# Attention values brought back to rows: three transposes, a copy and two GpSimd steps against one product and one VectorE step

## The chip, the cores and the metric

One core of a Trainium2 chip. It has five engines with a queue each: TensorE (PE; its weight loads are listed apart, as PEld), VectorE (DVE), ScalarE (ACT), GpSimd (POOL) and SyncE (SP, which here issues most of the transfers). They meet through semaphores only: an instruction adds to one when it has finished, and another engine waits for a count. PE writes to PSUM, in 8 banks; DVE and ACT read PSUM and SBUF; POOL reads and writes SBUF only. The metric is the time of one execution on the device, in microseconds (us).

## The reference

Three parts in a row, all in float32, for 2 batches of 768 rows:

```python
q_bits, k_bits = (q @ proj > 0), (k @ proj > 0)          # 6 hash bits a row
mask = bucket(q_bits)[:, None] == bucket(k_bits)[None, :]
scores = np.where(mask, scale * q @ k.T, -1e9)
attn = np.exp(scores - scores.max(-1))
out = attn / (attn.sum(-1) + 1e-9) @ v                   # 16 heads (2 x 8), 768 x 64 each
x = heads side by side                                   # (2, 768, 512)

u = x + real(fft2(x)); un = layernorm(u)                 # first mixer
x = u + relu(un @ w_ch1) @ w_ch2

theta = x @ w_theta                                      # second mixer
u = x + w_tok_r @ (x * cos(theta)) + w_tok_i @ (x * sin(theta))
out = u + relu(u @ w_ch)
```

## The kernel before

Every float32 matrix product is made of three products of rounded parts (high x high, high x low, low x high), so each operand exists as a high part (type fp32r, written by ACT or POOL) and a low part (the difference, by DVE or POOL). The plain float32 tensors that PE sees are the ones it transposes.

**Attention** runs over 16 heads `h` (`NH`) and, in each, over six tiles of 128 query rows, t = 0 to 5 (`QT`). `schedule()` writes the order out by hand as a list of slots, one for each tile; every engine's block walks the same list and takes its own share of a slot, so the order on each engine is fixed and only semaphores place it in time. In the slot of tile n:

- PE makes the scores of tile n (L1006, L1007, into one of two double banks), transposes the exponentials E of tile n - 2 in two units `eta` and `etb` of three 128x128 transposes (L981), adds a third of the value products of a half head (`pv`, L1021 and L1022, into the one bank `OT`), and then makes the slot's extra units: `bits` (hash bits of the next head, t = 0 and 1) or `back` (t = 3 and 5, for the head before). The units `eta`, `etb`, `bits` and `back` take turns in a ring of three banks; `take_bank` waits until the unit three back has been emptied.
- DVE takes the maximum of the scores (`negmax`, L1237), makes scale and bias for the exponential from it (`affine`, L1240, 128x2), writes the two low parts `ETL` (L1247), and in the slot t = 3 makes the reciprocals of the row sums (`einv`, L1266 and L1268).
- ACT writes the high parts `ETH` (L768), the exponential `E` (L775), the copy `OS` of a finished half head out of `OT` (L787), and the copies of the extra units (`MB` for bits, `OL` for back).
- POOL runs freely behind its semaphores: `mask_rows` (MR, L562; slot t = 1, when ACT has copied both bits units), `scale_q` (QK, L547) and `split_top` (the copy TOPH, L555, and TOPL, L557; t = 2), `split_v` (VHL, L581 and L583; t = 4), some folds for the transform in the last heads, and `finish`.

What the change touches is the way of the values back to rows. `OS` holds a half head transposed: 64 partitions of products with the high part of v and 64 with the low part, for 3 x 128 rows. Before, a `back` unit transposes it in three 128x128 pieces into a ring bank (L992), ACT copies the bank to `OL2` (L800), and POOL's `finish` adds the two halves of 64 columns into `OS2` (L571) and multiplies by `einv` into the rows of X (L574), for the first half in slot t = 3 of the next head and for the second in t = 0 of the one after:

```python
nc.gpsimd.tensor_tensor(OS2[:], OL2[:, i, :, 0:D], OL2[:, i, :, D:P], ALU.add)
nc.gpsimd.tensor_tensor(X[:, row:row + HALF, (h % H) * D:(h % H + 1) * D], OS2[:], einv..., ALU.mult)
```

The semaphore `s_x` counts the halves of X written; the folds for the transform, the first loads of the feed-forward weights and DVE's `fold_sum` (AE, L1156) wait for it.

After attention come the transform of X by matrix products (`half_transform`, `cosine_part`, `sine_part`), the feed-forward part (`hidden` and `shrink`, 48 steps) and the second mixer (`steps`). Of these the change only touches waits on PE.

Of the kernel before, what the change touches and what calls it, by code (L numbers as in the profile page):

```python
# [84 lines left out]
def program(nc, qk, v, projb, w1, w2, wth, wtr, wti, wch, ident_in, gamma_in, sign_in, cs_in, ss_in, alt_in, cd_in, sd_in, out):  # L85
# [16 lines left out]
    X = put("X", [P, NT, DM])  # L102
    ident = put("ident", [P, P])
    negmax = put("negmax", [P, NSTAT, 2])
    affine = put("affine", [P, NSTAT, 2])
# [12 lines left out]
    halfpi = put("halfpi", [P, 1])  # L118
    tail = used[0] + 4 * 2 * DM
    OL2 = put("OL2", [P, 2, HALF, P], F32, tail - 4 * 2 * DM)  # L120
    OS2 = put("OS2", [P, HALF, D])
    used[0] = tail
    tail = used[0]
# [112 lines left out]
    with ctx:  # L236
# [39 lines left out]
        for u in units:  # L276
# [30 lines left out]
                   "pv": sem("s_os"),  # L307
                   "back": sem("s_ol")}
        s_sum = sem("s_sum")
        s_x = sem("s_x")  # L310
        s_mr = sem("s_mr")
# [144 lines left out]
        def _(sp):  # L456
# [38 lines left out]
            load_qk(1)  # L495
            sp.dma_start(ident[:], ident_in).then_inc(s_ident, 16)
            move_away(0)
# [38 lines left out]
        def _(pool):  # L536
# [22 lines left out]
            def mask_rows(h):  # L559
                pool.wait_ge(emptied["bits"], 2 * (h + 1))  # L560
                pool.wait_ge(s_mask, 32 * h)
                nc.gpsimd.tensor_scalar(MR[:], MB[:], gamma[:, 0:1], gamma[:, 1:2], ALU.is_gt, ALU.mult).then_inc(s_mr, 1)  # L562

            def finish(h, i):
                half = 2 * h + i
                st = slice((half * HALF) % NSTAT, (half * HALF) % NSTAT + HALF)
                row = (h // H) * QT + i * HALF
                pool.wait_ge(emptied["back"], half + 1)
                if half:
                    pool.wait_ge(s_x, half)  # L570
                nc.gpsimd.tensor_tensor(OS2[:], OL2[:, i, :, 0:D], OL2[:, i, :, D:P], ALU.add).then_inc(s_sum, 1)  # L571
                pool.wait_ge(s_sum, half + 1)
                pool.wait_ge(s_inv, 2 * (h + 1))
                nc.gpsimd.tensor_tensor(X[:, row:row + HALF, (h % H) * D:(h % H + 1) * D], OS2[:],  # L574
                                        einv[:, st].unsqueeze(2).to_broadcast([P, HALF, D]), ALU.mult).then_inc(s_x, 1)

# [65 lines left out]
            for slot, (tile, et, pv, us) in enumerate(slots):  # L642
                h, t = divmod(slot - 1, QT)
                if slot and t == 0:
                    if h == 0:
                        split_top(1)
                        split_v(0)
                    elif h > 1:
                        finish(h - 2, 1)
                if slot and t == 1 and h + 1 < NH:  # L650
                    mask_rows(h + 1)
                if slot and t == 2 and h + 2 < NH:
                    scale_q(h + 2)
                    split_top(h + 2)
                if slot and t == 3 and h:
                    finish(h - 1, 0)
                if slot and t == 4 and h + 1 < NH:
                    split_v(h + 1)
                if slot and t in (2, 5) and early:
                    dst, src, landed = early.pop(0)  # L660
                    pool.dma_start(dst, src).then_inc(landed, 16)
                if (h, t) in ((9, 5), (10, 5), (11, 5)):
                    fold_part(h - 9, False)
                if (h, t) in ((12, 5), (13, 5), (14, 1)):
                    fold_part(h - 12, True)
                if (h, t) == (14, 2):
                    fold_even(0)
                if (h, t) == (14, 5):
                    fold_odd(0)
                if (h, t) == (15, 1):  # L670
                    fold_even_low(0)
                if (h, t) == (15, 4):
                    fold_odd_low(0)
            finish(NH - 1, 1)
            fold_odd(1)
# [32 lines left out]
        def _(act):  # L708
# [50 lines left out]
            for slot, (tile, et, pv, us) in enumerate(slots):  # L759
# [28 lines left out]
                for u in us:  # L788
                    kind, h, i = u
                    c = slice(i * HC, (i + 1) * HC)  # L790
                    if kind == "bits" and h:
# [3 lines left out]
                        nc.scalar.activation(MB[:, c], ring(unit_no[u])[0:2 * NM, 0:HC], ACT.Copy).then_inc(emptied["bits"], 1)  # L795
                    elif kind == "back":
                        act.wait_ge(s_ring, done[u])
                        if h:
                            act.wait_ge(s_sum, nth[u] - 2)
                        nc.scalar.activation(OL2[:, i], blocks(ring(unit_no[u])[:, 0:HC]), ACT.Copy).then_inc(emptied["back"], 1)  # L800
                    elif kind == "s1" and i < TG - 1:
                        half_high(0, i)
# [84 lines left out]
        def _(pe):  # L887
# [81 lines left out]
            def unit(name):  # L969
# [4 lines left out]
                if kind in ("eta", "etb"):  # L974
                    tile = h * QT + i
                    pe.wait_ge(s_exp, tile + 1)
                    if tile == 0:
                        pe.wait_ge(s_ident, 16)
                    first = 0 if kind == "eta" else HALF
# [9 lines left out]
                elif kind == "back":  # L989
                    pe.wait_ge(emptied["pv"], 2 * h + i + 1)  # L990
                    for j in range(HALF):
                        last = nc.tensor.transpose(bank[:, j * P:(j + 1) * P], OS[:, i, j * P:(j + 1) * P], ident[:])  # L992
                last.then_inc(s_ring, 1)

            for tile, et, pv, us in slots:
                if tile is not None:
                    h, t = divmod(tile, QT)
                    pe.wait_ge(s_away, 32 * (h + 1))
                    pe.wait_ge(s_in, 32 * (h + 1))
                    pe.wait_ge(s_mask, 32 * (h + 1))  # L1000
                    if tile >= 2:
# [10 lines left out]
                if pv is not None:  # L1012
                    h, c, part = pv
                    if part == 0:
                        pe.wait_ge(s_vs, 2 * h + 2)
                        pe.wait_ge(emptied["eta"], h * QT + (c + 1) * HALF)
                        pe.wait_ge(emptied["etb"], h * QT + (c + 1) * HALF)
# [44 lines left out]
            def hidden(g):  # L1062
                c, f = divmod(g, FT)
                pe.wait_ge(s_uth, CH * (c + 1))
                pe.wait_ge(s_utl, CH * (c + 1))
                if g >= 2:
# [37 lines left out]
            def step(kind, n, t):  # L1104
# [6 lines left out]
                elif kind in ("theta", "channel"):  # L1111
                    y = xt_no[kind, n]
                    pe.wait_ge(s_xth, y + 1)
                    pe.wait_ge(s_xtl, y + 1)
                    pe.wait_ge(s_wlow, n_wth if kind == "theta" else n_wch)
                    take_turn(kind, n)
# [4 lines left out]
                elif kind == "mix":  # L1121
                    c = n % QT
                    pe.wait_ge(s_zl, 2 * (n + 1))
                    pe.wait_ge(s_wlow, n_wth + 2 * (c + 1))
                    if n == 0:
# [24 lines left out]
        def _(dve):  # L1150
# [80 lines left out]
            for slot, (tile, et, pv, us) in enumerate(slots):  # L1231
# [22 lines left out]
                for u in us:  # L1254
# [6 lines left out]
                    elif kind == "s1" and i < 2:  # L1261
                        half_low(0, i)
                    elif kind == "back" and i == 0:
                        st = slice(h * QT % NSTAT, h * QT % NSTAT + QT)
                        dve.wait_ge(s_exp, (h + 1) * QT)
                        nc.vector.tensor_scalar(einv[:, st], esum[:, st], 1e-9, None, ALU.add).then_inc(s_inv, 1)  # L1266
                        dve.wait_ge(s_inv, 2 * h + 1)
                        nc.vector.reciprocal(einv[:, st], einv[:, st]).then_inc(s_inv, 1)  # L1268

# [147 lines left out]
def constants():  # L1417
# [6 lines left out]
    def parts(a):  # L1424
# [5 lines left out]
    return {  # L1430
        "ident": np.eye(P, dtype=np.float32),
        "gamma": np.array([[0, 1]] * BITS + [[-TINY, 1]] * BITS + [[-TINY, -PEN]] * BITS + [[0, -PEN]] * BITS, dtype=np.float32),
# [48 lines left out]
```

## Time and profile before

| | |
|---|---|
| median of 3 runs | 743.95 us (743.7 to 744.09) |
| the profiled execution | 744.51 us, its span 742.7 us |
| PE (matmul) busy | 716.0 us, 96% |
| PE weight loads | 604.6 us, 81% |
| DVE busy | 427.9 us, 58% |
| ACT busy | 336.6 us, 45% |
| POOL busy | 322.8 us, 43% |
| granted TensorE clock | 1.0 of full speed |

The span runs from the first instruction to the last; the time has some 1.8 us around it. The ends of matmuls are modelled and overlap, so a busy PE is not yet a PE at its peak: what matters is whether one starts as the one before lets it. Shares over the whole span hide that the stages differ: DVE is nearly always busy in attention and mostly idle behind it.

### The profile page before, as it was taken

What the parts mean: (1) busy time and instruction counts of PE and PEld (TensorE: products, weight loads), DVE (VectorE), ACT (ScalarE), POOL (GpSimd) and SP (SyncE); (2) the same over time, 40 slices, a digit from 0 to 9 for tenths busy, and PEclk for the clock granted to TensorE, in tenths of its full rate; (3) what the DMA queues carried; (4) which work ended last, traced back from release to release, by engine and by line L of the source; (5) the groups of instructions that cost most, each with busy time, mean ns of one, the idle gap of its engine ahead of it and who ended that gap; (6) DMA issues with size and microseconds to landing.
All of it is one profiled execution on the core that took longest, in us unless ns stands there. A gap on an engine that the chain in (4) does not pass through costs nothing.

```text
span 742.7 us, 10815 instructions
## 1 busy us (share of the span) xinstructions
PE 716.0 (96%) x3754; PEld 604.6 (81%) x3754; DVE 427.9 (58%) x731; ACT 336.6 (45%) x689; POOL 322.8 (43%) x284
## 2 busy tenths in 40 slices
PE   3999999999998999999999999999999999999998
PEld 2788888888887877788888888888888888888876
DVE  2899999999999777733122121211333556845443
ACT  1899989988987834433210111121223344123101
POOL 3688878878887339855100000020033564221100
PEclk9999999999999999999999999999999999999999
DMA  6464753444332012423000000110011210000002
GB/s 162 117 146 113 176 146 84 99 113 100 88 73 66 1 44 64 135 85 100 0 1 1 0 1 2 41 57 22 1 42 44 85 50 29 1 28 15 15 28 86
DMA packets 39399, 45.76 MB, mean 62 GB/s; under 512 B 15796, under 2 KB 26676, under 8 KB 39348
## 3 DMA queue, kind: packets, MB, share of 16 engines
q1 hardware_dynamic: 36564, 41.65, 20.5%
q0 software_dynamic: 2784, 3.43, 1.8%
q8 instruction: 32, 0.52, 0.3%
q14 instruction: 19, 0.16, 0.1%
HBM read 28.16 MB, written 3.15 MB: 42 GB/s over the span
## 4 chain that ended last, share of the span: by engine, by line
PE 76%; DVE 15%; issue 4%; ACT 2%; DMA 1%; POOL 1%; SPq 0%; ACTq 0%; POOLq 0%; DVEq 0%
PE PS L890 21%; PE PS L892 21%; PE PS L891 21%; DVE negmax L1237 6%; DVE ETL L1247 4%; DVE affine L1240 3%; PE PS L1021 2%; PE PS L981 2%; PE PS L1007 2%; PE PS L1006 2%; PE PS L1022 2%; PE PS L1109 1%; ACT OS L787 1%; PE PS L1036 1%; PE PS L992 1%
## 5 line engine op out<-in xcount | busy, mean ns | idle before, releaser
L1390 DVE SCALAR_TENSOR_TENSOR HL<-PS,HH 128x512 fp32r<-128x512 f32 x48 | 33.1, 691 | 154.7 <-ACT HH L876 154.7
L775 ACT ACTIVATE E<-PS,affine 128x768 f32<-128x768 f32 x96 | 95.2, 992 | 38.8 <-DVE affine L1240 36.1
L876 ACT ACTIVATE HH<-PS 128x512 fp32r<-128x512 f32 x48 | 28.7, 598 | 180.9 <-PE PS L892 180.9
L1237 DVE TENSOR_REDUCE negmax<-PS 128x1 f32<-128x768 f32 x96 | 90.8, 946 | 16.9 <-PE PS L1007 15.8
L1247 DVE TENSOR_TENSOR ETL<-PS,ETH 128x384 fp32r<-128x384 f32 x192 | 97.0, 545 | 2.5 <-ACT ETH L768 2.5
L981 PE MATMUL PS<-ident,E 128*128 128x128 f32 x576 | 81.8, 275 | 2.2 <-DVE ETL L1247 2.1
L768 ACT ACTIVATE ETH<-PS 128x384 fp32r<-128x384 f32 x192 | 82.7, 486 | 0.9 <-PE PS L981 0.8
L1021 PE MATMUL PS<-ETH,VHL 128*128 128x384 f32 x192 | 72.3, 377 | 5.2 <-ACT OS L787 4.7
L890 PE MATMUL PS<-UTH,W 128*128 128x512 f32 x192 | 75.8, 395 | 0.2 <-issue 0.2
L1006 PE MATMUL PS<-TOPH,TOPL 128*128 128x512 f32 x192 | 69.1, 360 | 6.5 <-DMA KM<-MR 6.2
L892 PE MATMUL PS<-UTH,W 128*128 128x512 f32 x192 | 74.8, 390 | 0.0
L891 PE MATMUL PS<-UTL,W 128*128 128x512 f32 x192 | 74.8, 389 | 0.0
L892 PE MATMUL PS<-W2H,HL 128*128 128x512 f32 x192 | 74.7, 389 | 0.0
L890 PE MATMUL PS<-W2H,HH 128*128 128x512 f32 x192 | 74.7, 389 | 0.0
L891 PE MATMUL PS<-W2L,HH 128*128 128x512 f32 x192 | 74.7, 389 | 0.0
L981 PEld LDWEIGHTS PS<-ident,E 128*128 128x128 f32 x576 | 65.4, 141 | 6.0 <-DVE ETL L1247 4.7
L1022 PE MATMUL PS<-ETL,VHL 128*128 128x384 f32 x192 | 64.7, 337 | 0.0
L693 POOL TENSOR_TENSOR WAL<-SRC,WAH 128x512 fp32r<-128x512 f32 x4 | 5.1, 1282 | 136.8 <-ACT WAH L852 136.8
L1007 PE MATMUL PS<-KM,QM 76*128 76x512 f32 x192 | 62.8, 347 | 0.0
L702 POOL TENSOR_TENSOR ZF<-X,SC 128x512 f32<-128x512 f32 x24 | 30.5, 1294 | 71.1 <-ACT SC L857 71.1
L562 POOL TENSOR_SCALAR MR<-MB,gamma 24x768 fp32r<-24x768 f32 x15 | 44.0, 2931 | 38.4 <-ACT MB L795 38.4
L890 PE MATMUL PS<-ZH,WTH 128*128 128x512 f32 x144 | 57.5, 400 | 0.0
(173 smaller groups left out, 1572.2 us busy)
## 6 DMA issues: line engine op xcount, KB each, us to landing
RAW<-in_moe_w_ch_dram SPq DMA_DIRECT2D x32, 256.0 KB, 2.7
QK<-in_qk_dram SPq DMA_DIRECT2D x16, 384.0 KB, 3.8
QM<-TOPH SPq DMA_DIRECT2D x16, 192.0 KB, 2.9
KM<-TOPL SPq DMA_DIRECT2D x16, 192.0 KB, 3.2
VR<-in_v_dram SPq DMA_DIRECT2D x16, 192.0 KB, 2.7
TOPL<-QM SPq DMA_DIRECT2D x16, 192.0 KB, 2.7
TOPH<-TOPH SPq DMA_DIRECT2D x16, 192.0 KB, 3.0
out_dram<-fin SPq DMA_DIRECT2D x12, 256.0 KB, 2.0
```

The source lines that it names most:

```text
L768: nc.scalar.activation(ETH[:, t // HALF, k * HALF:(k + 1) * HALF, (t % HALF) * P:(t % HALF + 1) * P], bank, ACT.Copy).then_inc(s_eth, 1)
L775: nc.scalar.activation(E[:, tile % NE, :], s_bank(tile)[:, 0:S], ACT.Exp, bias=affine[:, t, 1:2], scale=affine[:, t, 0:1], accum_out=esum[ ...
L890: nc.tensor.matmul(dst, hl, hr, start=start, stop=False)
L891: nc.tensor.matmul(dst, hl, lr, start=False, stop=False)
L892: return nc.tensor.matmul(dst, ll, hr, start=False, stop=stop)
L981: last = nc.tensor.transpose(bank[:, j * P:(j + 1) * P], E[:, tile % NE, (first + j) * P:(first + j + 1) * P], ident[:])
L1006: nc.tensor.matmul(dst, TOPL[:, h % 3, c], TOPH[:, h % 3, lo:hi], start=True, stop=False)
L1007: last = nc.tensor.matmul(dst, QM[:, h % 2, c], KM[:, h % 2, lo:hi], start=False, stop=True)
L1021: nc.tensor.matmul(OT, VHL[:, h % 2, j, :], ETH[:, c, j, :], start=(j == 0), stop=False)
L1022: last = nc.tensor.matmul(OT, VHL[:, h % 2, j, :], ETL[:, c, j, :], start=False, stop=(j == QT - 1))
L1237: nc.vector.tensor_reduce(negmax[:, t, 1:2], s_bank(tile)[:, 0:S], AX_X, ALU.max, negate=True).then_inc(s_max, 1)
L1247: nc.vector.tensor_tensor(ETL[where], blocks(ring(unit_no[kind, h, t])[:, 0:HC]), ETH[where].bitcast(F32), ALU.subtract).then_inc(emptied[ ...
```

## The change

- `ident` gets a companion `twins`, 128x64, two 64x64 identities on top of each other (one more load at the start, from columns 128 to 191 of the same constant).
- A `back` unit is three products of a piece of OS (128x128, as the weights) with `twins` (64 columns), which bring the piece back and add its two halves in one; all in plain float32.
- DVE multiplies the 3 x 64 columns in PSUM by `einv` straight into X, in the slot of the unit, for the first half behind the reciprocal. ACT's copy to `OL2` and POOL's `finish` go, and their semaphores; the ring bank is free when DVE has written X (`s_x` is now `emptied["back"]`).
- Waits of PE that repeat one already passed are dropped: per tile, per value group, per feed-forward step, per mixer step.

```diff
     ident = put("ident", [P, P])
+    twins = put("twins", [P, D])
     negmax = put("negmax", [P, NSTAT, 2])
...
                    "pv": sem("s_os"),
-                   "back": sem("s_ol")}
-        s_sum = sem("s_sum")
-        s_x = sem("s_x")
+                   "back": sem("s_x")}
+        s_x = emptied["back"]
         s_mr = sem("s_mr")
...
             load_qk(1)
-            sp.dma_start(ident[:], ident_in).then_inc(s_ident, 16)
+            sp.dma_start(ident[:], ident_in[:, 0:P]).then_inc(s_ident, 16)
+            sp.dma_start(twins[:], ident_in[:, P:P + D]).then_inc(s_ident, 16)
             move_away(0)
...
 
-            def finish(h, i):
-                half = 2 * h + i
-                st = slice((half * HALF) % NSTAT, (half * HALF) % NSTAT + HALF)
-                row = (h // H) * QT + i * HALF
-                pool.wait_ge(emptied["back"], half + 1)
-                if half:
-                    pool.wait_ge(s_x, half)
-                nc.gpsimd.tensor_tensor(OS2[:], OL2[:, i, :, 0:D], OL2[:, i, :, D:P], ALU.add).then_inc(s_sum, 1)
-                pool.wait_ge(s_sum, half + 1)
-                pool.wait_ge(s_inv, 2 * (h + 1))
-                nc.gpsimd.tensor_tensor(X[:, row:row + HALF, (h % H) * D:(h % H + 1) * D], OS2[:],
-                                        einv[:, st].unsqueeze(2).to_broadcast([P, HALF, D]), ALU.mult).then_inc(s_x, 1)
-
             def split_v(h):
...
                         nc.scalar.activation(MB[:, c], ring(unit_no[u])[0:2 * NM, 0:HC], ACT.Copy).then_inc(emptied["bits"], 1)
-                    elif kind == "back":
-                        act.wait_ge(s_ring, done[u])
-                        if h:
-                            act.wait_ge(s_sum, nth[u] - 2)
-                        nc.scalar.activation(OL2[:, i], blocks(ring(unit_no[u])[:, 0:HC]), ACT.Copy).then_inc(emptied["back"], 1)
                     elif kind == "s1" and i < TG - 1:
...
                     tile = h * QT + i
-                    pe.wait_ge(s_exp, tile + 1)
+                    if kind == "eta":
+                        pe.wait_ge(s_exp, tile + 1)
                     if tile == 0:
-                        pe.wait_ge(s_ident, 16)
+                        pe.wait_ge(s_ident, 16 * 2)
                     first = 0 if kind == "eta" else HALF
...
                     for j in range(HALF):
-                        last = nc.tensor.transpose(bank[:, j * P:(j + 1) * P], OS[:, i, j * P:(j + 1) * P], ident[:])
+                        last = nc.tensor.matmul(bank[:, j * D:(j + 1) * D], OS[:, i, j * P:(j + 1) * P], twins[:], start=True, stop=True)
                 last.then_inc(s_ring, 1)
 
             for tile, et, pv, us in slots:
                 if tile is not None:
                     h, t = divmod(tile, QT)
-                    pe.wait_ge(s_away, 32 * (h + 1))
-                    pe.wait_ge(s_in, 32 * (h + 1))
-                    pe.wait_ge(s_mask, 32 * (h + 1))
+                    if t == 0:
+                        pe.wait_ge(s_away, 32 * (h + 1))
+                        pe.wait_ge(s_in, 32 * (h + 1))
+                        pe.wait_ge(s_mask, 32 * (h + 1))
                     if tile >= 2:
...
                     if part == 0:
-                        pe.wait_ge(s_vs, 2 * h + 2)
-                        pe.wait_ge(emptied["eta"], h * QT + (c + 1) * HALF)
+                        if c == 0:
+                            pe.wait_ge(s_vs, 2 * h + 2)
                         pe.wait_ge(emptied["etb"], h * QT + (c + 1) * HALF)
...
                 c, f = divmod(g, FT)
-                pe.wait_ge(s_uth, CH * (c + 1))
-                pe.wait_ge(s_utl, CH * (c + 1))
+                if f == 0:
+                    pe.wait_ge(s_uth, CH * (c + 1))
+                    pe.wait_ge(s_utl, CH * (c + 1))
                 if g >= 2:
...
                     c = n % QT
-                    pe.wait_ge(s_zl, 2 * (n + 1))
-                    pe.wait_ge(s_wlow, n_wth + 2 * (c + 1))
+                    if t == (CH if n == 0 else 0):
+                        pe.wait_ge(s_zl, 2 * (n + 1))
+                        if n < QT:
+                            pe.wait_ge(s_wlow, n_wth + 2 * (c + 1))
                     if n == 0:
...
                         half_low(0, i)
-                    elif kind == "back" and i == 0:
-                        st = slice(h * QT % NSTAT, h * QT % NSTAT + QT)
-                        dve.wait_ge(s_exp, (h + 1) * QT)
-                        nc.vector.tensor_scalar(einv[:, st], esum[:, st], 1e-9, None, ALU.add).then_inc(s_inv, 1)
-                        dve.wait_ge(s_inv, 2 * h + 1)
-                        nc.vector.reciprocal(einv[:, st], einv[:, st]).then_inc(s_inv, 1)
+                    elif kind == "back":
+                        if i == 0:
+                            st = slice(h * QT % NSTAT, h * QT % NSTAT + QT)
+                            dve.wait_ge(s_exp, (h + 1) * QT)
+                            nc.vector.tensor_scalar(einv[:, st], esum[:, st], 1e-9, None, ALU.add).then_inc(s_inv, 1)
+                            dve.wait_ge(s_inv, 2 * h + 1)
+                            nc.vector.reciprocal(einv[:, st], einv[:, st]).then_inc(s_inv, 1)
+                            dve.wait_ge(s_inv, 2 * h + 2)
+                        half = h * QT + i * HALF
+                        st = slice(half % NSTAT, half % NSTAT + HALF)
+                        row = (h // H) * QT + i * HALF
+                        dve.wait_ge(s_ring, done[u])
+                        nc.vector.tensor_tensor(X[:, row:row + HALF, (h % H) * D:(h % H + 1) * D],
+                                                ring(unit_no[u])[:, 0:HALF * D].rearrange("p (a b) -> p a b", b=D),
+                                                einv[:, st].unsqueeze(2).to_broadcast([P, HALF, D]), ALU.mult).then_inc(s_x, 1)
 
...
     return {
-        "ident": np.eye(P, dtype=np.float32),
+        "ident": np.concatenate([np.eye(P), np.tile(np.eye(D), (2, 1))], axis=1).astype(np.float32),
         "gamma": np.array([[0, 1]] * BITS + [[-TINY, 1]] * BITS + [[-TINY, -PEN]] * BITS + [[0, -PEN]] * BITS, dtype=np.float32),
```

## Rows read from the trace of the kernel before

**Rows 1.** busy time by stage: stretch, length, each engine's busy us (instructions)

```profile
30.11:221.87 191.76, 188.27 (x1246) 169.84 (x1245) 181.44 (x339) 172.68 (x391) 158.75 (x143) 1.00 0.46 116
221.87:268.34 46.47, 42.53 (x263) 36.16 (x261) 36.29 (x66) 33.12 (x76) 23.49 (x27) 1.00 0.15 39
268.34:742.70 474.36, 468.67 (x2176) 386.69 (x2176) 196.06 (x302) 118.42 (x202) 125.04 (x96) 1.00 0.12 37
```

**Rows 2.** chain of waits in one head: start us, us, what

```profile
116.34 0.41 PE PS L1021
...
117.28 0.33 PE PS L992 x3
...
118.33 0.66 PE PS L981 x6
...
123.55 0.97 DVE negmax L1237
...
124.54 0.52 DVE affine L1240
125.06 0.93 DVE ETL L1247 x2
...
129.15 0.17 DVE affine L1240
...
130.43 0.39 ACT OS L787
...
130.95 0.41 PE PS L1021
```

**Rows 3.** timeline of POOL, 123.5 to 131.5 us: start us, us, engine, line, operation

```profile
124.08 2.93 POOL L562 TENSOR_SCALAR MR<-MB,gamma 24x768 fp32r<-24x768 f32 x1 [2.92 <-ACT MB L795]
126.99 2.13 POOL L547 TENSOR_SCALAR QK<-QK 64x768 f32<-64x768 f32 x1
129.19 0.82 POOL L555 CAST TOPH<-QK 128x768 fp32r<-128x768 f32 x1
130.09 1.83 POOL L557 TENSOR_TENSOR TOPL<-QK,TOPH 128x768 fp32r<-128x768 f32 x1
```

**Rows 4.** timeline of DVE in the same stretch

```profile
128.09 0.19 DVE L1268 RECIPROCAL einv<-einv 128x6 f32<-128x6 f32 x1
128.20 0.92 DVE L1237 TENSOR_REDUCE negmax<-PS 128x1 f32<-128x768 f32 x1
```

**Rows 5.** timeline of DVE, 59 to 62.5 us

```profile
60.42 0.42 DVE L1240 SCALAR_TENSOR_TENSOR affine<-negmax 128x2 f32<-128x2 f32 x1
```

**Rows 6.** timeline of POOL in the same stretch

```profile
60.31 0.51 POOL L581 CAST VHL<-VR 128x384 fp32r<-128x384 f32 x1
```

**Rows 7.** timeline of DVE, 104 to 107.5 us

```profile
107.01 0.49 DVE L1240 SCALAR_TENSOR_TENSOR affine<-negmax 128x2 f32<-128x2 f32 x1
```

**Rows 8.** timeline of POOL, 103 to 108 us

```profile
106.97 0.51 POOL L574 TENSOR_TENSOR X<-OS,einv 128x192 f32<-128x192 f32 x1
```

**Rows 9.** groups by line, 20 to 272 us: busy us, mean ns | idle before

```profile
L1247 DVE TENSOR_TENSOR ETL<-PS,ETH 128x384 fp32r<-128x384 f32 x192 | 97.0, 545 | 2.5 <-ACT ETH L768 2.5
...
L571 POOL TENSOR_TENSOR OS<-OL 128x192 f32<-128x192 f32 x32 | 19.2, 601 | 16.5 <-ACT OL L800 11.2 <-DVE einv L1268 5.0
...
L574 POOL TENSOR_TENSOR X<-OS,einv 128x192 f32<-128x192 f32 x32 | 16.3, 510 | 2.5
...
L992 PEld LDWEIGHTS PS<-ident,OS 128*128 128x128 f32 x96 | 12.4, 140 | 1.1
```

**Rows 10.** timeline of DVE, 295 to 299 us

```profile
296.92 0.41 DVE L1211 TENSOR_TENSOR DS<-PS,BS 128x257 f32<-128x257 f32 x1
297.25 0.41 DVE L1212 TENSOR_TENSOR DS<-PS,BS 128x257 f32<-128x257 f32 x1
```

**Rows 11.** timeline of DVE, end of attention

```profile
265.97 1.76 DVE L1156 TENSOR_TENSOR AE<-X 128x1536 f32<-128x1536 f32 x1 [1.18 <-POOL X L574]
```

**Rows 12.** timeline of PE, end of attention

```profile
268.34 0.42 PE L890 MATMUL PS<-SSH,OH 128*127 128x386 f32 x1 [0.63 <-DVE TL L1204]
```

More of the change, by code:

```diff
@@ L118, in program @@
     halfpi = put("halfpi", [P, 1])
[L119 to L122, printed above, removed]
+    used[0] += 4 * 2 * DM
     tail = used[0]
@@ L647, in _ @@
                         split_v(0)
-                    elif h > 1:
-                        finish(h - 2, 1)
                 if slot and t == 1 and h + 1 < NH:
@@ L654, in _ @@
                     split_top(h + 2)
-                if slot and t == 3 and h:
-                    finish(h - 1, 0)
                 if slot and t == 4 and h + 1 < NH:
@@ L673, in _ @@
                     fold_odd_low(0)
-            finish(NH - 1, 1)
             fold_odd(1)
@@ L1114, in step @@
                     pe.wait_ge(s_xtl, y + 1)
-                    pe.wait_ge(s_wlow, n_wth if kind == "theta" else n_wch)
+                    if n == 0:
+                        pe.wait_ge(s_wlow, n_wth if kind == "theta" else n_wch)
                     take_turn(kind, n)
```

## The prediction

> **What bounds the kernel now.** I read the stages first, then the chain of waits inside one head, then the two engines that the change shifts work between.
>
> The stages [rows 1]: the 13 heads from 30.11 to 221.87 us take 191.76 us, 14.75 each; the last two heads and the run out of attention take 46.47; the transform, the feed-forward part and the second mixer take 474.36, of which PE is busy 468.67. In the third stretch PE is fed without gaps, so a wait that is dropped there was over when PE came to it. The attention heads are the place to look: PE busy 188.27 and DVE 181.44 of 191.76, POOL 158.75.
>
> There the chain of waits alternates [rows 2]. From 116.34 to 123.55 it runs on PE alone: one group of value products, one "back" unit (three transposes, 0.33), then scores, transposes and value products of the next tiles. From 123.55 to 129.32 it runs on DVE alone, tile t=2 to t=4 of the head: maximum, affine, two ETL pieces, and again, with the two small einv operations between. The affine of t=4 then releases the exponential on ACT, ACT copies OS at 130.43, and PE, which has only one bank OT for value products, goes on at 130.95. So a head is 14.61 here, and whatever is put on DVE between t=2 and t=4 is paid in full; PE and ACT have no part of it that could hide it.
>
> The same stretch on POOL [rows 3] and DVE [rows 4] shows what DVE waits for. The affine at 124.54 is 0.52 long instead of 0.16 and ends 0.98 after POOL began MR at 124.08. The next ones are free, and the one of t=4 starts at 129.15, 0.04 before POOL begins its copy into TOPH at 129.19. Both engines are timed from the start of MR (POOL runs MR, QK, TOPH, TOPL without a gap; DVE runs on from the release of the affine), so this phase repeats in nearly every head. What the copy does to an affine that comes later can be read elsewhere [rows 5, 6]: the affine at 60.42 met a POOL copy of the same kind (CAST, 60.31 to 60.82) and ended at 60.84, held to the copy's end. An affine at 107.01 met the multiplication into X and was held to 107.50 [rows 7, 8]. Heads with that hold are longer than 14.61; over the 13 heads such holds cost 191.76 - 13 x 14.61 = 1.8 us.
>
> **What the change removes.** POOL loses OS and X, 32 x (0.601 + 0.510) = 35.5 us [rows 9]. POOL is not what ends the wait in a head: MR waits 2.92 us for ACT [rows 3], and the operations behind MR are chained to MR. What comes back are the holds by these operations on the affine, the 1.8 us above. ACT loses the 32 copies into OL; before the affine of t=4 ACT is waiting anyway, so nothing comes back. The repeated waits on PE: in the PE stretch the groups follow each other without a gap [rows 2], in the last stage too [rows 1]: nothing. If they do cost something there, PE's idle of 191.76 - 188.27 = 3.5 us bounds it.
>
> **What it adds on PE.** A "back" unit becomes three products with 64 columns instead of three transposes with 128. No plain f32 product is in this trace. Below: half the columns of the transposes, 0.16 a unit. Above: each product done as two, each with a load of its own at the pace of a transpose (0.66 / 6 = 0.11, [rows 2]), 0.66 a unit. The weights loaded are the same 128x128 OS as before, with loads of 140 ns [rows 9]; I stay with that row, 0.33, no change. Only one of the head's two units is in the PE stretch (the other, in slot t=3, runs while DVE sets the pace), so the ends are 14 x (-0.17) = -2.4 and 14 x 0.33 = +4.6 us. The Trainium skill (FP8 and Floating Point Precision, TensorE Precision Notes) says that a true FP32 product takes four passes; no row here shows it, and by it 64 columns at 2.4 GHz would be 0.107 us a product, an estimate that leaves the unit at 0.32 and the sum as it is.
>
> **What it adds on DVE.** 32 multiplications, 128x192, one operand in PSUM and einv from SBUF. Nearest rows: the DS operations (257 elements, PSUM and SBUF) start 0.33 apart [rows 10], two ETL pieces of 384 take 0.93, 0.465 each [rows 2]; the line through both gives 0.27 for 192. In slot t=3 it comes behind the reciprocal and now waits for it: today the maximum starts at 128.20, inside the reciprocal's 128.09 to 128.28 [rows 4]; the multiplication can start at 128.30 and the maximum at 128.57. That is 0.37 later. The product that it reads was done long before. (The one in slot t=5 falls where DVE waits for PE's scores: nothing.) The ETL pieces average 545 ns over 192 [rows 9], the time of one that runs free, so an operation with one operand in PSUM is not held by POOL; I take the multiplication as not held either.
>
> **What is late next.** The affine of t=4 would start at 129.52 instead of 129.15. It then falls into the copy into TOPH, 129.19 to 130.01 [rows 3], and by [rows 5, 6] ends just behind it, at 130.03, instead of 129.31: 0.72 late, twice what was added. Exponential, OS copy and PE follow it, so the head becomes 14.61 + 0.72 = 15.33. POOL's TOPL from 130.09 holds the affine of t=5 to about the same time as before, and behind it PE sets the pace again, so nothing more is added.
> Which part of a POOL instruction holds the affine decides this. MR, 2.93 long, let it go after 0.98 [rows 2, 3]; the CAST kept it to its end. The Trainium skill (SBUF — State Buffer, Who interferes with whom) says that a DVE instruction with two SBUF inputs contends with a GpSimd one that reads SBUF, and that the one that comes first has the shared ports for the whole instruction. By that rule the copy holds the affine as the CAST row has it, and the sum is the one below; MR's row does not agree with it, and by MR's row alone the copy would let the affine through (the second rival).
>
> **The sum.** 13 heads: 13 x 15.33 - 191.76 = +7.5 (the holds that go away are in it). The end: the last X now comes from DVE instead of ACT and POOL; today DVE's AE waits 1.18 for it and PE then 0.63 for a TL behind it [rows 11, 12]; PE gets the 0.63 back, -0.6. The last two heads: POOL's folds run earlier without the X work and meet other affines, and two multiplications are added. Ends: -3.9 (all of PE's idle there, 46.47 - 42.53 [rows 1]) and +2.6 (2 x 0.37 and one hold as long as TOPL's 1.83 [rows 3]); I take 0 between them. Start: the second table load is issued in SP's idle time before the first move, nothing. Together +6.9, on the profiled execution's 744.51 (span 742.7 and 1.8 around it) 751.4; the runs' median is 743.95, 0.56 below it, so 750.9.
>
> **Rivals.**
> 1. The forecast with a dear product: 0.66 a unit on PE, 4.6 more, 755.5. For it: nothing in the trace shows an f32 product. Against: the same loads, half the columns.
> 2. The copy into TOPH holds only at its start, as MR does (0.98 / 2.93 of 0.82 is 0.27; the affine comes 0.33 in). Then a head is 14.61 + 0.37 and 13 x 14.98 - 191.76 - 0.6 = +2.4: 746.4. Against it stands the CAST row.
> 3. The other side: MR comes earlier. If the OL copies taken from ACT let MB, and so MR, start 0.9 earlier against DVE, the affine of t=2 is free (0.36 back, which pays the multiplication), the copy into TOPH is over when the affine of t=4 comes, a head is 14.61 and 13 x 14.61 - 191.76 - 0.6 = -2.4: 741.5. It decides from 0.9 us on; against it, ACT's MB follows an exponential that follows PE's scores, and the copy taken away lies a tile earlier.
> 4. The held affine of t=4 loses to TOPL as well (130.09 to 131.92): 1.9 more a head, +25, 776. Against: the gap of 0.08 between them, in which a waiting instruction is first.
>
> **How the numbers follow.** The forecast with a product at up to about 0.5 has 0.50, rival 1 0.13, rival 2 0.17, rival 3 0.09, rival 4 0.05; 0.06 is for what I don't see, spread over all signs. What a measurement here can tell from no change is about 0.2%, 1.5 us. Faster: rival 3 and a little, 0.11. Same: the low part of rival 2 (with the product's low end) and a little, 0.08. Slower: 0.81. The range takes the forecast with the ends of the product and of the last heads (748 to 754), rival 1 and most of rival 2: 745 to 757.
>
> **What would show it.** DVE: 32 multiplications near 0.35; the affine of t=4 near 0.5, ending with the copy into TOPH; affines of t=0 and t=1 near 0.16. Heads near 15.3 apart. PE: "back" units near 0.33, and longer waits for the OS copy. POOL some 35 us less busy, ACT 15. No change behind 300 us but the shift. Wrong would make it: an affine of t=4 that stays at 0.16, MR that starts earlier against the maximum of t=2, a product above 0.2 each, or a multiplication that POOL holds.

## The result, and the profile after

The changed kernel takes 760.7 us (median; 760.21 to 761.39), the kernel before 743.92 beside it: ratio 1.0225, 95% interval 1.0213 to 1.0237. It is slower by 16.8 us; 750.9 was forecast, in a range from 745 to 757 that does not hold it. The profiled execution has a span of 758.6 us (before 742.7).

The stages, in the form of [rows 1]: stretch, length, then each engine's busy us (instructions) in the order PE, PEld, DVE, ACT, POOL, then the granted clock and, last, the DMA engines' busy share and GB/s.

```profile
29.70:233.13 203.43, 195.99 (x1324) 179.51 (x1323) 178.18 (x365) 166.18 (x366) 133.88 (x96) 1.00 0.44 110
233.13:284.26 51.13, 47.38 (x280) 41.49 (x279) 38.39 (x72) 30.71 (x66) 13.77 (x10) 0.93 0.12 34
284.26:758.60 474.34, 468.68 (x2177) 386.67 (x2176) 196.07 (x302) 118.88 (x203) 125.05 (x96) 1.00 0.12 37
```

The 13 heads are 11.67 longer (203.43 against 191.76), the last two heads with the run out of attention 4.66 (51.13 against 46.47), the rest is as long as before, and the start is 0.41 shorter. That is 15.9, the whole difference of the spans.

The chain of waits in one head of the changed kernel, as in [rows 2] (start us, us, what):

```profile
128.77 0.97 DVE negmax L1218
...
129.77 0.51 DVE affine L1221
130.27 0.93 DVE ETL L1228 x2
...
133.53 0.36 DVE X L1256
133.89 0.88 DVE negmax L1218
...
134.79 0.46 DVE affine L1221
...
136.35 0.39 ACT OS L767
...
136.88 0.41 PE PS L998
...
137.82 0.61 PE PS L968 x6
138.43 0.29 PE PS L983
```

The stretch on DVE, from the maximum of t=2 to the end of the affine of t=4, took 5.77 before (123.55 to 129.32) and takes 6.48 (128.77 to 135.25): the multiplication (L1256) is in it, and the affine of t=4 is 0.46 long instead of 0.17. Behind OS, the three products of a unit (L968, six records) take 0.61 where the three transposes took 0.33 [rows 2], and the first score product behind them 0.29 where it took 0.24. Its line of the kernel before, in the same chain:

```profile
117.61 0.24 PE PS L1006
```

The timeline of POOL beside it, as in [rows 3], shows what the affine waited for: it ended at 135.25, just behind the copy into TOPH (134.40 + 0.82 = 135.22).

```profile
129.29 2.93 POOL L560 TENSOR_SCALAR MR<-MB,gamma 24x768 fp32r<-24x768 f32 x1 [6.24 <-ACT MB L775]
...
134.40 0.82 POOL L553 CAST TOPH<-QK 128x768 fp32r<-128x768 f32 x1
135.31 1.84 POOL L555 TENSOR_TENSOR TOPL<-QK,TOPH 128x768 fp32r<-128x768 f32 x1
```

Groups by line, 20 to 290 us, as in [rows 9] (busy us, mean ns | idle before): each product is two loads and two matmuls (32 units x 3 products = 96, in 192 records), and the multiplication takes 357 ns.

```profile
L968 PEld LDWEIGHTS PS<-twins,OS 128*128 128x128 f32 x192 | 26.6, 194 | 0.0
L968 PE MATMUL PS<-twins,OS 128*128 128x64 f32 x192 | 25.4, 269 | 0.0
...
L1256 DVE TENSOR_TENSOR X<-PS,einv 128x192 f32<-128x192 f32 x32 | 11.4, 357 | 6.1 <-PE PS L968 5.6
```

At the end of attention DVE's AE no longer waits, as it did in [rows 11]; the timeline of DVE:

```profile
281.14 0.35 DVE L1256 TENSOR_TENSOR X<-PS,einv 128x192 f32<-128x192 f32 x1
281.62 1.76 DVE L1137 TENSOR_TENSOR AE<-X 128x1536 f32<-128x1536 f32 x1
```

In head 14 something else happens. PE alone, one microsecond a row: stretch, length, busy us (records), granted clock, DMA.

```profile
246.00:247.00 1.00, 0.32 (x3) 1.00 0.55 163
247.00:248.00 1.00, 0.46 (x3) 1.00 0.02 8
248.00:249.00 1.00, 0.43 (x3) 1.00 0.00 0
249.00:250.00 1.00, 1.00 (x7) 0.68 0.00 0
250.00:251.00 1.00, 1.00 (x5) 0.50 0.00 0
...
255.00:256.00 1.00, 1.00 (x5) 0.50 0.00 0
256.00:257.00 1.00, 1.00 (x9) 0.90 0.00 0
```

For three microseconds PE is idle more than half of the time; then the granted clock falls from 1.00 to 0.50 (2.4 to 1.2 GHz) until some 256. Ahead of it DVE was held twice by POOL's folds (timelines of DVE, then of POOL; an affine or an einv that nothing holds takes 0.16). The first of these holds, in slot 3, was there before as well and as long (1.00), with the clock at 1.00 throughout:

```profile
242.04 1.00 DVE L1221 SCALAR_TENSOR_TENSOR affine<-negmax 128x2 f32<-128x2 f32 x1
...
243.90 1.11 DVE L1248 TENSOR_SCALAR einv<-esum 128x6 f32<-128x6 f32 x1
```

```profile
241.76 1.26 POOL L575 TENSOR_TENSOR AO<-X 128x512 f32<-128x512 f32 x1
243.16 1.81 POOL L579 TENSOR_TENSOR FE<-AE 128x765 f32<-128x765 f32 x1
```

### The profile page after: what moved, and what is told of

Same layout as the page of the kernel before. It is cut to its first block, busy times and chain, and to the rows that moved or that the text cites. A ratio compares the mean times of both kernels' runs of the same rounds, so it can differ in the third digit from the quotient of the medians.

```text
span 758.6 us, 10450 instructions
## 1 busy us (share of the span) xinstructions
PE 728.7 (96%) x3850; PEld 619.7 (82%) x3850; DVE 426.8 (56%) x763; ACT 328.1 (43%) x657; POOL 288.1 (38%) x220
## 4 chain that ended last, share of the span: by engine, by line
PE 79%; DVE 15%; issue 3%; ACT 1%; DMA 1%; SPq 0%; ACTq 0%; DVEq 0%
PE PS L865 21%; PE PS L867 21%; PE PS L866 20%; DVE negmax L1218 6%; DVE ETL L1228 4%; PE PS L998 3%; DVE affine L1221 3%; PE PS L957 3%; PE PS L983 3%; PE PS L984 2%; PE PS L999 2%; PE PS L968 1%; PE PS L1087 1%; ACT OS L767 1%; DVE X L1256 1%
```

## The experiments

One table first, to which each experiment refers. It cuts each profiled span in four: to the first maximum of head 1, from there to the first maximum of head 14, on to DVE's AE, and the rest. Each row is one profiled execution; the median is that of all runs. The period of a head is the time from its first maximum to that of the next.

```
                                   start  heads 1-13  to AE   rest    span   median
before                             30.11    191.76    44.10  476.73  742.7   743.92
changed                            29.70    203.43    48.49  476.98  758.6   760.7
e1 waits dropped, else before      29.31    191.71    44.11  476.77  741.9   744.7
e2 changed, with transposes        30.24    199.03    44.61  476.72  750.6   754.24
e3 before, with the products       30.00    203.46    44.79  476.95  755.2   756.93
e4 changed, query split first      29.56    206.51    45.61  477.02  758.7   760.41
e5 changed, unit in slot 4         29.86    192.26    43.47  477.01  742.6   744.37
e6 changed, folds late             29.28    203.30    44.76  477.06  754.4   757.21
e7 before, unit in slot 4          29.38    189.91    43.16  476.75  739.2   741.13
e8 e7 with folds late              29.42    189.86    43.82  476.80  739.9   742.05
e9 e5 with folds late              30.09    192.25    43.77  477.09  743.2   744.67
e10 e5 with rounded products       29.23    189.60    42.78  476.79  738.4   740.92
```

The medians of the kernel before that stand beside the experiments are 744.09 to 744.38, and the ratios are taken against those. The start lies between 29.23 and 30.24 with no order by kernel, the rest between 476.72 and 477.09. The first stretch is therefore not read.

**e1, the dropped waits alone, on the kernel before.** Edits of this kind at six places; one of them:

```diff
-                    pe.wait_ge(s_away, 32 * (h + 1))
-                    pe.wait_ge(s_in, 32 * (h + 1))
-                    pe.wait_ge(s_mask, 32 * (h + 1))
+                    if t == 0:
+                        pe.wait_ge(s_away, 32 * (h + 1))
+                        pe.wait_ge(s_in, 32 * (h + 1))
+                        pe.wait_ge(s_mask, 32 * (h + 1))
```

> The kernel before with the repeated waits of PE dropped and nothing else. Theory: a wait on a count that was reached long ago costs nothing that the trace shows, so the median stays at 743.9 within 0.2% (742.5 to 745.4). Rival: the waits cost PE's issue something in the long stages, and dropping them gains 1.5 or more; then the change hides a gain and its other parts cost more than the 16.8 by which it is slower.

Measured: 744.7, ratio 1.0005 (0.9996 to 1.0014); heads, last heads and the rest are within 0.1 of before. The waits cost nothing that can be measured (0.14% at most), and the change hides no gain in them.

**e2, the changed kernel with transposes.**

```diff
-  last = nc.tensor.matmul(bank[:, j * D:(j + 1) * D], OS[:, i, j * P:(j + 1) * P], twins[:], start=True, stop=True)
+  last = nc.tensor.transpose(bank[:, j * P:(j + 1) * P], OS[:, i, j * P:(j + 1) * P], ident[:])
...
-  ring(unit_no[u])[:, 0:HALF * D].rearrange("p (a b) -> p a b", b=D),
+  blocks(ring(unit_no[u])[:, 0:HC])[:, :, 0:D],
```

> The changed kernel with the three transposes of 128x128 in place of the three products with the twins; VectorE multiplies the high 64 columns of each block alone, so the low half of the value products is left out of the sum. Theory (the products are dear: a unit's three take 0.61 on the chain and the scores behind them 0.05 more, against 0.33 for the transposes): each head of 1 to 13 loses 0.34, so the period goes from 15.66 to about 15.32, 13 heads give back about 4.4, and with the last heads the time is 755 to 757. Rival (the products are hidden and the collision of the affine with the POOL copy is all of the 1.05 a head): the time stays at 760.7 within 1.5.

Measured: 754.24, ratio 1.0141 (1.0121 to 1.0161), a little under the expected range. The heads are 15.30 to 15.35 apart, as the theory had it, and 4.40 shorter than the changed kernel's; they are still 7.27 longer than before. The rival is out. The rest of the gain is in the last heads, 3.88: the profiled execution kept its clock there, though PE's idle before that is much the same as in the changed kernel:

```profile
242.00:243.00 1.00, 0.45 (x4) 1.00 0.62 185
243.00:244.00 1.00, 0.33 (x3) 1.00 0.02 8
244.00:245.00 1.00, 0.43 (x3) 1.00 0.00 0
245.00:246.00 1.00, 1.00 (x8) 1.00 0.00 0
```

The folds hold DVE in it as they do in the changed kernel: slots 3 and 4 of head 14, from maximum to maximum, are 4.48 and 2.31 long against 4.47 and 2.33. Only behind them do the two differ, in the last slot of head 14 (2.82 against 4.40) and the first of head 15 (2.08 against 3.85), which is 3.35 of the 3.88. Some 0.33 of it is the product in the last slot; the other 3.0, by that estimate, is what PE loses at 0.50. Of e2's four runs two have spans of 750.6 and 750.7 (mean clock 0.999 and 1.000) and two 753.1 and 753.3 (0.998). e4 below has such idle too (PE busy 0.26, 0.54 and 0.43 from 249 to 252) and keeps 1.00 there. Such idle therefore goes with a fall in some executions and not in others.

**e3, the products alone, on the kernel before.** PE as in the change; ScalarE copies the sums, POOL only multiplies:

```diff
-  last = nc.tensor.transpose(bank[:, j * P:(j + 1) * P], OS[:, i, j * P:(j + 1) * P], ident[:])
+  last = nc.tensor.matmul(bank[:, j * D:(j + 1) * D], OS[:, i, j * P:(j + 1) * P], twins[:], start=True, stop=True)
...
-  nc.gpsimd.tensor_tensor(OS2[:], OL2[:, i, :, 0:D], OL2[:, i, :, D:P], ALU.add).then_inc(s_sum, 1)
```

> The kernel before with the product with the twins alone: ScalarE copies the 192 columns to SBUF as before and POOL multiplies as before, but no longer adds; VectorE is given nothing new. Theory (the product costs 0.33 a unit on the chain that sets the head's period): 13 heads by 0.34 is +4.4, less what POOL's missing additions give back to the affines, so 746 to 749. Rival (the product is dear only together with the multiplication on VectorE): 743.9 within 1.

Measured: 756.93, ratio 1.0169 (1.0155 to 1.0183), outside both expectations. The heads take 203.46, as long as with the whole change, although DVE has no multiplication. The timelines of DVE and of POOL in head 7 show what holds it:

```profile
134.89 0.67 DVE L1238 SCALAR_TENSOR_TENSOR affine<-negmax 128x2 f32<-128x2 f32 x1
```

```profile
134.73 0.82 POOL L555 CAST TOPH<-QK 128x768 fp32r<-128x768 f32 x1
```

The affine of t=4 comes 0.16 behind the start of the copy (slot 3 of this head is 2.44 long, 2.28 to 2.29 before: the maximum of t=4 now waits for its scores, which PE makes behind the product) and is held for 0.67. The sum of slots 3 and 4 (from the maximum of t=3 to that of t=5) is 4.95 to 5.00 in the changed kernel, in e2 and in e3, against 4.24 or 4.25 before: the affine's end is pinned to the end of the copy, whatever made it late. So either half of the change alone costs some 0.72 a head here, and both cost it once; the product's 0.33 in slot 5 (3.14 against 2.81) comes on top wherever there is a product.

**e4, the query of head h+2 split ahead of the mask rows.**

```diff
-                if slot and t == 1 and h + 1 < NH:
-                    mask_rows(h + 1)
-                if slot and t == 2 and h + 2 < NH:
-                    scale_q(h + 2)
-                    split_top(h + 2)
+                if slot and t == 1:
+                    if h and h + 2 < NH:
+                        scale_q(h + 2)
+                        split_top(h + 2)
+                    if h + 1 < NH:
+                        mask_rows(h + 1)
```

> The changed kernel with POOL's scaling and splitting of the query of head h+2 issued ahead of the mask rows of head h+1, so that the copy into TOPH is over before the affine of slot 4. Theory (the affine of slot 4 is held to the end of that copy, mean 0.456 where 0.16 is the free price): the period falls by 0.30, from 15.66 to about 15.36, and the time to about 756.8, if the copy and the difference behind it don't hold the affines of slots 1 and 2 instead. Rival (the length of the affine is hidden, and the period is PE's): the period stays at 15.66 and the time at 760.7.

Measured: 760.41, ratio 1.0216 (1.0202 to 1.023). Both are right in part. The affine of t=4 is free in heads 1 to 13 (0.16), and heads 10 to 13 have a period of 15.39 to 15.43, as expected. But in heads 7 to 9 the copy's successor TOPL now holds the affine of t=0 (timelines of DVE and of POOL), those heads are 16.3 long; heads 1 and 2 take 17.41 and 16.85, with the clock at 0.50 from about 46 to 49. Why DVE and PE stand still ahead of that fall was not followed. The collision was moved, not removed.

```profile
126.47 1.62 DVE L1225 SCALAR_TENSOR_TENSOR affine<-negmax 128x2 f32<-128x2 f32 x1
```

```profile
126.23 1.84 POOL L555 TENSOR_TENSOR TOPL<-QK,TOPH 128x768 fp32r<-128x768 f32 x1
```

**e5, the changed kernel with the first half's unit a slot later.**

```diff
-        if h and t in (3, 5):
-            units.append(("back", h - 1, t // 5))
+        if h and t in (4, 5):
+            units.append(("back", h - 1, t - 4))
```

> The changed kernel with the first half's unit brought back in slot 4 instead of slot 3, so that the reciprocals (0.30) and the multiplication (0.36) come behind the affine of slot 4 and that affine runs before POOL's copy into TOPH. Theory (the stretch of VectorE from slot 2 to the affine of slot 4 sets the head together with PE): the period falls from 15.66 by 0.30 for the held affine and up to 0.66 for what leaves the stretch, less what the product now adds in slot 4: 14.9 to 15.3, so 750 to 756. Rival (PE's own work of two products is the bound once they are there): the period stays within 0.1 of 15.66, and the time at 759 to 761.

Measured: 744.37, ratio 1.0006 (0.9996 to 1.0015): with one slot changed the whole loss is gone, more than the theory gave (750 to 756, and a period of 14.9 to 15.3, not 14.80). The affine of t=4 starts before the copy into TOPH and is 0.16 long again (timelines of DVE and of POOL), and PE, with two dear units in slots 4 and 5, is never idle in these heads (stretches, columns as above):

```profile
128.98 0.16 DVE L1221 SCALAR_TENSOR_TENSOR affine<-negmax 128x2 f32<-128x2 f32 x1
```

```profile
129.28 0.82 POOL L553 CAST TOPH<-QK 128x768 fp32r<-128x768 f32 x1
```

```profile
30.00:120.00 90.00, 90.00 (x620) 83.76 (x619) 82.91 (x171) 78.24 (x173) 64.12 (x49) 1.00 0.58 140
120.00:220.00 100.00, 100.00 (x690) 93.52 (x689) 92.57 (x190) 86.77 (x191) 66.91 (x44) 1.00 0.38 95
```

Its period, 14.80 to 14.82 from head 2 on, is thus PE's own work with the products. On the chain two units take 2 x 0.33 more than two of transposes; but e7 below, with transposes in these slots, is only 0.2 a head shorter.

**e6, the changed kernel with two folds of head 14 later.**

```diff
-                if (h, t) in ((12, 5), (13, 5), (14, 1)):
+                if (h, t) in ((12, 5), (13, 5), (14, 5)):
                     fold_part(h - 12, True)
-                if (h, t) == (14, 2):
-                    fold_even(0)
                 if (h, t) == (14, 5):
+                    fold_even(0)
                     fold_odd(0)
```

> The changed kernel with POOL's two folds of head 14 issued behind the split of the last head's values, so that they no longer hold VectorE's affine and reciprocals in slots 3 and 4 of that head. Theory (PE stands idle there because VectorE is held, and the granted clock, 0.69 from 250 to 260 in the changed kernel, falls after that): the clock stays at 1.00 and the last two heads lose 2.5 to 4.5, so 756 to 758.2. Rival (the clock falls for another reason, or the folds hold something later instead): 760.7 within 1.5.

Measured: 757.21, ratio 1.0175 (1.016 to 1.019), as the theory had it. The stretch from head 14 to AE goes from 48.49 to 44.76, and the clock is 1.00 in it.

```profile
240.00:260.00 20.00, 17.32 (x116) 15.60 (x114) 18.71 (x33) 15.24 (x34) 11.34 (x9) 1.00 0.12 31
```

**e7 and e8, the kernel before with the unit in slot 4, and with the folds late too.** The edits of e5, and of e5 and e6, on the kernel before.

> The kernel before with the first half's unit and its reciprocals in slot 4 instead of slot 3. Theory (VectorE's stretch from slot 2 to the affine of slot 4 sets the head): it is 0.30 shorter without the reciprocals, and 13 heads give 739 to 742. Rival (the reciprocals only move to the next stretch, which is just as tight, or TOPL's difference holds slot 5's affine longer): 743.9 within 1.5, or slower.

Measured: 741.13, ratio 0.9964 (0.9951 to 0.9977). The heads lose 1.85 rather than 13 x 0.30: the period is 14.53 to 14.62 in ten of them, and the chain through head 7 now runs on PE almost without a break (PE busy 188.66 of the 189 us from 30 to 219, 185.81 before). With DVE's stretch shorter, PE is next; its transposes of E take up to 0.86 a six there instead of 0.66, and what holds them was not followed.

> The kernel before with the first half's unit in slot 4 and with POOL's two folds of head 14 behind the split of the last head's values. Theory: the folds held slot 3's affine of head 14 for 1.00 instead of 0.16 and made that head 17.65 long against 14.6 to 14.9 for the others; 1 to 3 of it come back on top of the first edit: 736 to 741. Rival (the folds then hold the last head instead): the same as the first edit alone.

Measured: 742.05, ratio 0.9974 (0.9963 to 0.9985): the rival. Head 14 is 14.48 instead of 15.72, and the last head gives it back: the folds hold its affines of t=0 and t=2 (1.30 and 1.19), and the clock falls behind an idle of PE (PE alone, one microsecond a row):

```profile
239.00:240.00 1.00, 0.00 (x0) 1.00 0.00 0
240.00:241.00 1.00, 0.55 (x3) 1.00 0.00 0
241.00:242.00 1.00, 0.45 (x3) 1.00 0.00 0
242.00:243.00 1.00, 1.00 (x4) 0.50 0.00 0
```

**e9 and e10, on the kernel of e5.** e9 adds the late folds. e10 has the products on fp32r operands:

```diff
-    OS = put("OS", [P, 2, HC])
+    OS = put("OS", [P, 2, HC], F32R)
...
+                    nc.gpsimd.tensor_copy(twinsR[:], twins[:]).then_inc(s_ident, 1)
...
-  OS[:, i, j * P:(j + 1) * P], twins[:], start=True, stop=True)
+  OS[:, i, j * P:(j + 1) * P], twinsR[:], start=True, stop=True)
```

> The changed kernel with both edits tried one at a time before: the first half's unit in slot 4, and POOL's two folds of head 14 behind the split of the last head's values. In the kernel with the unit in slot 4 alone TensorE is busy all the time in heads 2 to 13 (period 14.80) and head 14 takes 16.46. Theory: head 14 comes down towards 14.8 and 1 to 2 are gained: 742.5 to 743.5. Rival: the folds hold the last head instead, as they did in the kernel before with both edits, and the time stays at 744.4 or rises.

Measured: 744.67, ratio 1.0009 (1.0 to 1.0019): the rival again. Head 14 is 16.73 (16.46 in e5); the folds hold the affine of slot 5 instead (1.68).

> The changed kernel with the unit in slot 4 and with the products of the twins on operands rounded to fp32r (ScalarE writes OS in fp32r and the twins are copied into an fp32r tile once), so the value products lose their low bits before they are turned. Theory: the price of a product is that an fp32 one is run as two loads and two matmuls (3 products are 6 records of each kind); as one of each, a unit takes about half of 0.61, TensorE's need of a head falls from 14.80 by 0.5 to 0.6, and with what VectorE's stretch then leaves the period is 14.3 to 14.6: 737 to 741. Rival: the loads of the 128x128 blocks set the price whatever their type is split into, and the period stays at 14.80: 744.4 within 1.

Measured: 740.92, ratio 0.9955 (0.9938 to 0.9972), in the range of the theory: one load and one matmul a product (groups by line), 0.25 a unit on the chain instead of 0.61, and a period of 14.48 to 14.72. The first score product behind the unit takes 0.32, though, not 0.24 (chain of waits), so a unit with it costs 0.57, as much as one of transposes (0.33 + 0.24), and 0.90 with plain f32 (0.61 + 0.29). e7, e8 and e10 are the versions that beat the kernel before; e10 pays with the low bits of the value products.

```profile
L974 PEld LDWEIGHTS PS<-twinsR,OS 128*128 128x128 f32 x96 | 15.1, 189 | 0.1
L974 PE MATMUL PS<-twinsR,OS 128*128 128x64 f32 x96 | 13.3, 248 | 0.0
```

```profile
126.88 0.25 PE PS L974 x3
127.13 0.32 PE PS L989
```

## Why the prediction was wrong

**The bound and the mechanism in the heads were right.** The heads are set by the chain that alternates between PE and DVE, the multiplication lies in it between t=2 and t=4, and the affine of t=4 then falls into the copy into TOPH and is held to its end. The affine of t=4 is 0.40 later against the maximum of t=3 (slot 3 is 2.68 long, 2.28 or 2.29 before; 0.37 forecast), of which the multiplication is 0.36 (0.27 forecast; the line through its two rows gives 0.26). It is held to the end of the copy in all 13 heads, and in e2, which has this half of the change without the product, the heads are 7.27 longer; +7.5 was the forecast. Rival 2 (the copy holds only at its start) and rival 4 (TOPL holds too) are out in the changed kernel, rival 3 (MR earlier) as well: in head 7 MR starts 0.48 before the affine of t=2 (129.29 and 129.77), in the kernel before 0.46 [rows 2, 3].

**The step that failed first is the product's term.** "I stay with that row, 0.33, no change", from the loads of the transposes [rows 9]. A unit takes 0.61, and the scores behind it 0.05 more: 0.66, the upper bound and the price of rival 1. Against e2 it costs the heads 203.43 - 199.03 = 4.40, which is 13 x 0.34; the bound said 14 x 0.33. The heads are thus those of rival 1, which had 0.13; its 755.5 still lacks the next step. A load of the f32 product is 194 ns long, not the 140 of [rows 9], and there are two for each product. The row of the transposes was the nearest by its tile, not by what PE does with it. The Trainium skill (FP8 and Floating Point Precision, TensorE Precision Notes) says four passes for true FP32; the trace shows two loads and two matmuls for each product and 0.61 / 3 = 0.20 us, not the 0.107 that was estimated by it. That estimate counts the columns alone, and they do not set the price here: a product of e10, one load and one matmul, still takes 0.25 / 3 = 0.08, where a quarter of the estimate is 0.03.

**The second is the last two heads: "I take 0 between them".** From head 14 to AE it is +4.39, beyond the bound of +2.6 even with the -0.6 at the end left out. That bound had added work and one hold; it had no row for a fall of the granted clock, since it is 1.00 in all three stretches of [rows 1]. e6 puts 3.73 of it down to the folds that hold DVE in slots 3 and 4 of head 14, together with the clock that falls behind them; e2's profiled execution, with the folds where they were and no fall, is 3.88 shorter, most of it in the slots where the clock is 0.50. Why the clock falls in all four runs of the changed kernel (mean 0.995 or 0.996), and why the mean is lower in two of e2's four, was not settled.

**Small terms.** The end: AE and PE no longer wait, as forecast, but PE still had work queued there, and the rest of the span is 0.25 longer, not 0.6 shorter. The waits on PE, ACT's copies and POOL's work: nothing, as forecast (POOL 322.8 to 288.1 us busy, the 35 named; ACT 336.6 to 328.1, 8.5 where 15 was named). The heads with holds by POOL's X work are gone, as forecast: the periods of the changed kernel are 15.64 to 15.69 from head 2 on.

**The sum by what was measured:** -0.41 (start) + 7.27 (multiplication and held affine, less the holds that went) + 4.40 (products) + 4.39 (last heads, mostly the clock) + 0.25 = 15.9, which is 758.6 - 742.7. One thing this order hides: by e3 the products alone would have cost the whole 11.7, since they push the same affine into the same copy.

The Trainium skill (SBUF — State Buffer, Who interferes with whom) calls the ports that VectorE and GpSimd share an exclusive lock and says, beside VectorE's two-port modes, "Whoever issues first gets the shared pair for the whole instruction". The copy into TOPH (the affine 0.46 long, 0.67 in e3) and TOPL in e4 (1.62) agree; MR lets the affine go after 0.99 of its 2.93 here too, which that rule does not explain. That ports are the cause is not shown here; the runs show only when the affine ends.

## What to carry to other kernels

Where an operation escapes a collision by a few hundredths of a microsecond, the cost of a delay is not the delay but a step: 0.16 late (e3) and 0.39 late (the change) in head 7 cost the same 0.72 here, because the end of the held instruction is pinned to the other engine. Look for such near misses first, and try the slot next to it: the same change with one unit a slot later is as fast as the kernel before, and the kernel before gains 0.4% by the same move. Against that one (741.13) the change in its better slot (744.37) still loses. When nothing in a trace does what an edit adds, take the bounds for real and give the dear one its full weight, above all where the nearest row is of another operation, as the transposes were here.

## What the runs showed of the hardware

- A product of a 128x128 f32 block with 64 f32 columns is two loads (194 ns each) and two matmuls, 0.20 us in a row of three; with both operands in fp32r it is one of each and 0.08 (e10). A f32 transpose of the same block takes 0.11 (0.33 for three). The 512-column matmul behind the three takes 0.29, 0.32 and 0.24.
- The granted clock fell from 1.00 to 0.50 behind three rows of 1 us in which PE was busy for 0.32, 0.46 and 0.43 (changed kernel), stayed there for about 7 us of unbroken PE work, and came back; after the like (0.45, 0.33, 0.43) in e2's profiled execution it did not fall. In e8 it was 0.50 from 242 to 245 only.
